# Six buffers for the first pieces of weights, their low halves placed later, and the fifth attention unit moved by three steps

## Time and profile before

| what | before |
|---|---|
| median of three runs | 1343.7 us |
| the profiled execution | 1343.41 us |
| its span (first to last instruction) | 1341.7 us |
| TensorE busy | 1325.3 us, 99% of the span |
| VectorE busy | 863.7 us, 64% |
| ScalarE busy | 602.0 us, 45% |
| GpSimd busy | 574.1 us, 43% |
| mean granted TensorE clock | 0.997 of full |

### The profile page before, as it was taken

How to read it: one execution, slowest core, us unless ns; L and a number is a source line. 1 busy time by engine, 2 the same in 40 slices (tenths; PEclk the granted TensorE clock), 3 DMA queues, 4 the chain that set the end, 5 groups by cost and what they waited for, 6 DMA issues and landing times.

```text
span 1341.7 us, 23409 instructions
## 1 busy us (share of the span) xinstructions
PE 1325.3 (99%) x8187; PEld 1298.7 (97%) x8187; DVE 863.7 (64%) x1681; ACT 602.0 (45%) x1227; POOL 574.1 (43%) x575
## 2 busy tenths in 40 slices
PE   8899999999999999999999999999999999999998
PEld 7799999999999999999999999999999999999998
DVE  8776556656543333346777687777777776777765
ACT  4544434434332222344445654545554446454541
POOL 4442212313115767224444644445644447544441
PEclk9999999999999999999999999999999999999999
DMA  6543223222202434212222333332243322342221
GB/s 166 158 113 65 67 45 67 62 50 67 54 10 93 126 111 125 89 57 95 84 88 77 89 100 125 96 95 77 89 130 95 94 75 73 115 126 89 88 65 48
DMA packets 80166, 118.77 MB, mean 89 GB/s; under 512 B 8112, under 2 KB 61872, under 8 KB 80048
## 3 DMA queue, kind: packets, MB, share of 16 engines
q1 hardware_dynamic: 80048, 117.26, 30.6%
HBM read 100.58 MB, written 14.55 MB: 86 GB/s over the span
## 4 chain that ended last, share of the span: by engine, by line
PE 94%; DVE 1%; issue 1%; DMA 1%; ACT 1%; ACTq 0%; DVEq 0%; SPq 0%
PE bank L1677 12%; PE bank L1679 11%; PE bank L1678 11%; PE bank L1878 10%; PE bank L1879 10%; PE bank L1880 10%; PE bank L1772 8%; PE bank L1774 7%; PE bank L1773 7%; PE bank L1642 2%; PE bank L1672 2%; PE bank L1651 1%; PE bank L1665 1%; PE bank L1850 1%; PE bank L1849 1%
## 5 line engine op out<-in xcount | busy, mean ns | idle before, releaser
L1148 POOL TENSOR_TENSOR wu<-w_r,wu 128x640 fp32r<-128x640 f32 (+1 forms) x132 | 200.7, 1524 | 323.0 <-ACT wu L881 323.0
L1878 PE MATMUL bank<-wd,h_hi 128*128 128x384 f32 x768 | 259.7, 338 | 0.0
L1879 PE MATMUL bank<-wd,h_hi 128*128 128x384 f32 x768 | 257.7, 335 | 0.0
L1880 PE MATMUL bank<-wd,h_lo 128*128 128x384 f32 x768 | 257.2, 335 | 0.0
L1500 DVE SCALAR_TENSOR_TENSOR xt<-bank,pn,xt 128x384 f32<-128x384 f32 x288 | 177.0, 615 | 97.3 <-PE bank L1880 88.4
L908 ACT ACTIVATE h_hi<-h 128x384 fp32r<-128x384 f32 x240 | 124.7, 524 | 196.5 <-DVE h L1450 80.0
L1772 PE MATMUL bank<-x_hi,wu 128*128 128x384 f32 x600 | 202.0, 337 | 2.4 <-ACT h L896 1.4
L1774 PE MATMUL bank<-x_lo,wu 128*128 128x384 f32 x600 | 202.7, 338 | 0.0
L1773 PE MATMUL bank<-x_hi,wu 128*128 128x384 f32 x600 | 200.9, 335 | 0.0
L1677 PE MATMUL bank<-xs_hi,wab 128*128 128x384 f32 x576 | 196.1, 340 | 1.5 <-ACT xs_hi L867 1.3
L1678 PE MATMUL bank<-xs_hi,wab 128*128 128x384 f32 x576 | 193.2, 336 | 0.0
(11 more groups left out here) (137 smaller groups left out, 2494.0 us busy)
## 6 DMA issues: line engine op xcount, KB each, us to landing
w_r<-weight_sums SPq DMA_DIRECT2D x120, 320.0 KB, 2.9
raw<-w SPq DMA_DIRECT2D x48, 576.0 KB, 4.0
unit<-fkq SPq DMA_DIRECT2D x62, 216.0 KB, 4.2
v_in<-v_chunks SPq DMA_DIRECT2D x32, 144.0 KB, 3.9
out<-xt SPq DMA_DIRECT2D x24, 192.0 KB, 4.4
weight_sums<-w_s SPq DMA_DIRECT2D x10, 384.0 KB, 4.4
xt<-ystage SPq DMA_DIRECT2D x48, 72.0 KB, 2.2
weight_sums<-w SPq DMA_DIRECT2D x40, 64.0 KB, 2.7
```

Of the source, the lines that this page charges most:

```text
L1148: eng.tensor_tensor(wu_piece(g, n, 1), wu_raw(g, n), wu_piece(g, n, 0).bitcast(f32), ALU.subtract).then_inc(s_ulo, 1)
L1878: eng.matmul(o, hh, w_hi, start=(f == fs[0]), stop=False)
L1879: eng.matmul(o, hh, w_lo, start=False, stop=False)
L1880: mm = eng.matmul(o, hl, w_hi, start=False, stop=(f == fs[-1]))
```

## The change

What it does, part by part:

- Pieces 0 to 5 of the first weights get a buffer each (`raw_x`, in the place of the x halves of the second block, and `raw_w`, in that of the low down weights). Their loads wait for nothing and are issued at the start, ahead of unit 4's; the two old buffers take pieces 6 and on. The loads of 6 and 7 are placed at step -3, behind the store of unit 2.
- The high halves of pieces 0 to 6 move from steps -14, -13, -11, -9, -7, -5, -4 to -11, -10, -8, -7, -5, -4, -1. The low halves were at the same steps; now they have steps of their own, in the order 0, 1, 3, 4, 2, 5, 6: piece 0 at -7; 1, 3 and 4 at -4 behind the states of unit 3; 2 at -2; 5 and 6 at -1.
- Unit 4 and all later ones move by three steps. The load of unit 4 is at the start as before, that of unit 5 is at step -9 (before: -6). Unit 4's `ends` moves by one step more.
- The splits of x for block 0 are at -3, -2, -1 (before -3, -1, -1); for block 1 at 31, 32, 33 (before 29, 31, 33), and they wait for the low halves of the first six pieces, whose buffers they take.
- The splits of the last three pieces of down weights move by three steps.
- Idle products: 2 before a turn instead of 5, 3 before each kv of units 0 to 3, 8 instead of 15 before the first up tile, and 6 within it, between tiles 0 and 1 of x and tile 2, behind a wait for the copy of unit 3's y.

The core of the diff:

```diff
-    WARM_UP, AT_TURN, AT_FFN = 35, 5, 15
+    WARM_UP, AT_TURN, AT_KV, AT_FFN, AT_X = 35, 2, 3, 8, 6
...
-    J = [APART * (u - FIRST - 1) for u in range(FIRST)] + [PACE * (u - FIRST) + 2 for u in range(FIRST, NU)]
+    J = [APART * (u - FIRST - 1) for u in range(FIRST)] + [PACE * (u - FIRST) + 5 for u in range(FIRST, NU)]
...
-    NEXT = dict(APART_FROM, limit=-7, logs=-6, sums=-5, decays=-4, gates=-4, ends=-3, keys=-2)
+    NEXT = dict(APART_FROM, load=-20, limit=-7, logs=-6, sums=-5, decays=-4, gates=-4, ends=-2, keys=-2)
...
     def split_at(r):
...
-            return J[0] + 1 + 9 * r // 5
-        return 2 * (r - R0)
+            return J[0] + (4, 5, 7, 8, 10, 11, 14)[r]
+        return 2 * (r - R0) + (3 if PIECES_1[r][0] == 2 and PIECES_1[r][2] * OPR >= FT1 // 2 else 0)
...
+    LOW_ORDER = (0, 1, 3, 4, 2, 5)
+    EARLY = len(LOW_ORDER)
+    LOW_AT = (J[0] + 8, J[0] + 11, J[0] + 13, J[0] + 11, J[0] + 11, J[0] + 14) + tuple(split_at(r) for r in range(EARLY, R1))
...
     def x_at(n, k):
-        return (-3, -1, -1)[k] if n == 0 else 36 * (n - 1) + (29 if n == 1 else 20) + 2 * k
+        return k - 3 if n == 0 else 31 + k if n == 1 else 36 * (n - 1) + 20 + 2 * k
...
+        early = ExitStack()
+        sb(early, "to_xs_hi11", [128, attn_bytes // 4 + 2 * KT * TB1])
+        raw_x = sb(early, "raw_x", [128, EARLY // 2, PIECE])
+        sb(early, "to_wo_lo", [128, 4 * KT * F1 + FT1 * DM])
+        raw_w = sb(early, "raw_w", [128, EARLY // 2, PIECE])
+        early.close()
...
+        s_early = [sem(f"s_early{n}") for n in range(EARLY)]
...
         def loaded_1(r):
...
-            return raw[:, r % 2, :].rearrange("p (f n) -> p f n", n=n)
-        def raw_loaded(r):
-            return 16 * (r // 2 + 1)
+            return raw_place(r).rearrange("p (f n) -> p f n", n=n)
+        def raw_place(r):
+            if r < EARLY:
+                return (raw_x, raw_w)[r // (EARLY // 2)][:, r % (EARLY // 2), :]
+            return raw[:, r % 2, :]
+        def raw_loaded(eng, r):
+            if r < EARLY:
+                eng.wait_ge(s_early[r], 16)
+            else:
+                eng.wait_ge(s_raw[r % 2], 16 * ((r - EARLY) // 2 + 1))
...
         def split_done(eng, r):
...
-            eng.wait_ge(s_wlo, r + 1)
+            eng.wait_ge(s_wlo, (LOW_ORDER.index(r) if r < EARLY else r) + 1)
...
         def split_free(eng, r):
...
         def x1_free(eng, n):
...
+            else:
+                eng.wait_ge(s_wlo, EARLY)
...
         def group(g):
...
             def load_raw(r):
-                if r >= 2:
+                if r >= EARLY + 2:
...
-                dst = raw[:, r % 2, :]
+                dst = raw_place(r)
...
-                eng.dma_start(dst, src).then_inc(s_raw[r % 2], 16)
+                eng.dma_start(dst, src).then_inc(s_early[r] if r < EARLY else s_raw[r % 2], 16)
...
             def load_w1(q):
...
             load_raw(0)
             load_raw(1)
             load_v(2)
+            load_raw(2)
+            load_raw(3)
+            load_v(3)
+            load_raw(4)
+            load_raw(5)
             load_unit(4)
-            load_v(3)
...
             for j in range(BEGIN, 3 * N1):
                 if j == STRONG_AT:
...
                 if (u := at(j, "store")) is not None:
...
-                if (u := at(j, "load")) is not None and u > FIRST:
+                if j == J[0] + 6:
+                    load_unit(FIRST + 1)
+                if (u := at(j, "load")) is not None and u > FIRST + 1:
                     load_unit(u)
                 if (u := at(j, "v")) is not None and u >= VRING:
                     load_v(u)
-                if j - 1 in SPLIT_AT and SPLIT_AT[j - 1] + 2 < R1:
+                if j == J[2] + 6:
+                    load_raw(EARLY)
+                    load_raw(EARLY + 1)
+                if j - 1 in SPLIT_AT and EARLY + 2 <= SPLIT_AT[j - 1] + 2 < R1:
                     load_raw(SPLIT_AT[j - 1] + 2)
                 if j == SUMS_AT - 3:
...
             def split_hi(r):
-                eng.wait_ge(s_raw[r % 2], raw_loaded(r))
+                raw_loaded(eng, r)
                 split_free(eng, r)
...
-                if j in SPLIT_AT and SPLIT_AT[j] < R0:
-                    first_lo(SPLIT_AT[j])
+                for r in sorted(range(R0), key=(LOW_ORDER + (EARLY,)).index):
+                    if j == LOW_AT[r]:
+                        first_lo(r)
...
                     if j == x2_at(n) - 1:
...
             def first_up_1():
...
+                    if ks[0]:
+                        eng.wait_ge(s_ys, FIRST)
+                        idle(SETS[1][0], AT_X)
                     for m in range(2):
                         for k in ks:
...
-            def idle(count):
+            def idle(to, count):
...
-                    eng.matmul(bank[3][:, 0:128], ident[:, :], ident[:, :], start=True, stop=True)
+                    eng.matmul(to[:, 0:128], ident[:, :], ident[:, :], start=True, stop=True)
...
-            idle(WARM_UP)
+            idle(bank[3], WARM_UP)
...
                     if i == 0 and part == 0:
-                        idle(AT_FFN)
+                        idle(bank[3], AT_FFN)
...
                 if (u := at(j, "turn")) is not None:
...
-                        idle(AT_TURN)
+                        idle(bank[3], AT_TURN)
                     turn(u)
                 if (u := at(j, "output")) is not None:
...
                 if (u := at(j, "scores")) is not None:
...
                 if (u := at(j, "kv")) is not None:
+                    if u < FIRST:
+                        idle(bank[3], AT_KV)
                     kv(u)
                 if j == CMIN_AT:
...
```

## The result

| | before | changed |
|---|---|---|
| median us | 1343.36 (13 runs, 1342.98 to 1343.78) | 1346.41 (13 runs, 1345.35 to 1348.14) |
| ratio | | 1.0023, 95% interval 1.0016 to 1.0031 |
| span of the profiled execution | 1341.7 | 1345.2 |

The changed kernel is slower by 3.1 us. The forecast was 1342.7, with 1346.2 as the upper end of the range and 0.12 for slower by over 0.2%: it was wrong in sign and in size.

What follows compares the result with a forecast made beforehand. TensorE, holding 94% of the chain of waits, was taken as the bound, with gains only before 60 us: first down product -2.0, unit 4's turn and kv +1.0, net -1.0 from 1343.7 to 1342.7 us; range 1339.0 to 1346.2.

Steps and rivals of the forecast that it cites:

- Upstream of the third tile: First block, attention's end: third x tile's products start at 41.75 instead of 46.38, 4.6 us earlier (bounds 3.0 and 6.0).
- The limit on the gates: Fourth unit's VectorE limit on gate logits, 0.94 long: begun 0.85 earlier it meets the same GpSimd instruction, ending as before.
- The store of the third y: Third unit's y, issued at 33.0: lands by 36.5 (37.9 by the slow row), three pieces, 2.1 each as unloaded.
- The queue behind it: VectorE after x's third low half: two low halves, sums, limit, gate at 46.9; TensorE loses 2.2, then 0.6 before scores.
- VectorE has keys of unit 4 ahead of the low half of h: Before the first down tile: low half of h at 50.1 if free, 51.5 behind a GpSimd split; 51.5 taken.
- the mark: First product of the first down tile: moves from 53.60 to 51.6 us, -2.0 (bounds 48.6 and 53.5).
- the slower rival: New TensorE gaps in the first block drop the clock; two falls on dense products give 1345.9, three 1347.5; chance 0.16.
- I cost this at nothing: Later attention units moved three steps, second block's x loaded at step 31: no cost, up to 1 us if cover fails.
- The idle products: Idle matmuls around the second x tile, 2.2 and 1.7 us: hidden under the two y stores with 0.4 to spare.
- 0.1 less was owed: Unit 4's turn and kv, done before the first down product until now, come after it: +1.0.
- the forecast's own -1.0: Net change of the whole kernel: -2.0 at the first down product, +1.0 for unit 4's turn and kv after it.
- the signs of being wrong: Scans of 1.05; 0.50 clock after 45; y store over 3.5; TensorE idle from 60 to middle; third unit's outputs before 32.5.

Runs made afterwards that it cites:

- experiment 2: Changed kernel with GpSimd's split of weight piece 8 waiting for the first low half of h: 1342.36 us, ratio 0.9992.
- experiment 3: Changed kernel with only GpSimd's split of piece 9 waiting, for unit 4's keys on VectorE: 1344.27 us, ratio 1.0005.
- experiment 9: Changed kernel with eleven idle products before the first down tile and the weight sums three steps earlier: 1343.21 us, ratio 1.0000.
- experiment 1: Changed kernel with the weight sums three steps earlier, at the step the kernel before had: 1345.20 us, ratio 1.0013.
- experiment 6: Kernel before the change, with its weight sums three steps later and nothing else: 1345.26 us, ratio 1.0018.
- experiment 4: Changed kernel with eleven idle products on TensorE before the first down tile: 1344.93 us, ratio 1.0013.
- experiment 5: Changed kernel with weight sums three steps earlier and GpSimd's split of piece 8 behind the first low half of h: 1341.03 us, ratio 0.9984.
- experiment 7: Changed kernel with unit 4, all later units and the weight sums at their old steps: 1341.08 us, ratio 0.9983.
- experiment 8: Changed kernel, weight sums earlier, split 8 waiting, low half of piece 5 and unit 4's sums before x's third low half: 1338.67 us, ratio 0.9967.

## Why the prediction was wrong

- **Upstream of the third tile it was right, and a little short.** The fourth y was copied at 35.6 (forecast 37.0), the third tile's products came at 40.50 (41.75). The limit on the gates did meet GpSimd (0.85 long) but cost 0.9 less than feared, so the outputs of the third unit ended at 31.4 instead of 32.5. (One sum of the forecast is off by 0.1: 33.0 + 1.2 + 2.2 is 36.4 and not 36.5; nothing depends on it.) The store of the third y landed in 1.9 to 2.0 and that of the fourth, behind two loads of weights, in 2.5 to 2.7. That is 0.5 more than in the earlier trace rows, not the 1.6 to 2.1 more of the earlier trace rows. The two loads had been issued 2.3 and 1.6 us ahead of the store, in the kernel before 1.6 and 0.4. That each engine takes its descriptors in ring order, as the Trainium skill says (DMA: Bandwidth & Descriptors, Queues, rings and completion order), fits with both, but the lead was not varied alone.
- **The queue behind it was right until 46.9.** Scans of 2.65 (2.68 forecast), a wait of 1.86 ahead of the second b tile (2.2), of 0.50 ahead of the scores (0.6).
- **The step that failed first** is "VectorE has keys of unit 4 ahead of the low half of h [...] 50.1 if free, 51.5 if the next GpSimd split is in the way". I gave each VectorE instruction one GpSimd instruction to wait for, the most that the rows at 46.66 and 51.63 show. The keys waited for three, the second gate and the splits of pieces 8 and 9 (4.88 instead of the 0.55 that they take alone); the upper bound of 53.5 held the mark, but the value taken was 0.8 short. Experiments 2 and 3 settle that GpSimd's run was the cause; why these keys lost three times in a row where other instructions lost once they do not tell.
- **The largest error is the clock.** It was the slower rival, at 0.16. I argued that the first fall would be hidden under the wait for the gates and asked for two falls. One fall, behind the last gap, lasted 6.8 us, twice the 3.2 of the earlier trace rows, and lay on dense products: 2.5. Filling the gap takes back 2.0 (experiment 9 against 1).
- **"I cost this at nothing"** was said of the phase of later steps, and I looked at the start of the second block only. The move also shifted what is placed from the last unit (the weight sums) against what is placed from the end of the layer. It cost 1.3 (experiment 1), and 1.95 put into the kernel before (experiment 6).
- The idle products cost nothing, as forecast: 0.95 of waiting was left behind them.

From the forecast's own -1.0: the mark came 0.8 later and 0.1 less was owed, so -0.3; with +2.5 for the clock and +1.4 for the gap that is +3.6, and the spans differ by 3.5. Of the signs of being wrong that the forecast named, three came: a clock of 0.50 after 45 us, idle time between 60 us and the middle, and the third unit's outputs well before 32.5.

## What to carry to other kernels

When a step is moved, list everything that is placed relative to it, to the end of the program, and everything that is not; the two meet somewhere. When two engines can hold each other up, look not only at the one instruction beside the victim but at how many are ready in a row behind it, because it may have to wait for all of them; a wait that breaks the run in front of the instruction that the bottleneck needs cost one line here and gave 4 us. And a gap in TensorE's work ahead of dense products is to be priced with the fall of the clock that may follow it.

## What the runs showed of the hardware that was not expected

- A VectorE multiplication of two SBUF tensors (0.56 alone) lasted 1.35, 3.14 and 4.88 us with one, two and three GpSimd instructions left to run when it started. GpSimd was hardly slowed there (1.82 and 2.03 for a split). The Trainium skill (GPSIMD Engine Reference, Key points) says that the two share SBUF interfaces for instructions with two SBUF inputs. These runs add that the one that waits can be starved, but more often gets in after one instruction: the low half of h at 51.63 in the kernel before waited for one (1.87), and the next GpSimd instruction took 1.32 instead of 1.00. The gate, which reads PSUM, was not held up: 0.54 at 55.48 in the kernel before, beside a GpSimd split that ran from 55.30 to 57.27.
- The granted clock fell to 0.50 in gaps of 3.52, but also, in some executions and not in others, behind one of 1.85. It stayed there for 6.8 us in the changed kernel (1.08 of the stretch from 50 to 52, all from 52 to 56, 1.72 of 56 to 58), where the earlier trace rows show about 3.2; in the profiled execution of experiment 1, after the same gap of 3.52, it stayed there for 3.4. What decides whether it falls behind a gap of 1.85, and for how long, was not settled.
- The time spreads over 2 to 4 us in the changed kernel and in experiments 2 to 4, 6 and 9, and over 0.7, 0.2 and 1.0 in experiments 5, 7 and 8. The falls of the clock are one source. The gap at 547 us is another: all of these but experiment 9 have it, and at full clock it was 0.23, 0.43, 1.14, 1.79 and 2.36 us long in the profiled executions of experiments 3 and 4, the changed kernel, experiments 6 and 2. Experiment 1, without it, still spreads over 1.7. What sets its length from one execution to the next was not looked into.
